# The first layer of block 0 in two 256-token sets, the first of them beside the second half of block 0's attention

## The reference

```python
# attention: batch 4, 8 heads, 768 steps, head size 48; w is the decay of every step
for t in range(S):
    cur = einsum('bhd,bhe->bhde', u * k[t], v[t])
    y[t] = einsum('bhd,bhde->bhe', r[t], state + cur)
    state = w[t][:, :, :, None] * state + einsum('bhd,bhe->bhde', k[t], v[t])
x = y.transpose(0, 2, 1, 3).reshape(3072, 384)
# first layer, d_ff 1536
x = (sigmoid(x @ w_gate) * (x @ w_val)) @ w_out
# second layer, d_ff 2048
h = x @ w2_in
out = where(h > 0, h, exp(min(h, 0)) - 1) @ w2_out
```

## Time and profile before

| | |
|---|---|
| runs shown | 1202.12, 1203.12, 1210.94 us (median 1203.12) |
| the profiled execution, first to last instruction | 1203.3 us |
| TensorE busy | 1155.1 us, 96% |
| VectorE, ScalarE, GpSimd busy | 669.5, 472.2, 295.5 us |
| mean granted TensorE clock | 0.987 |

### The profile page before, as it was taken

The page is one execution under the profiler, slowest core; times in us unless marked ns, Lnnn a source line. Parts: engine busy times, 40 slices in busy tenths (PEclk is TensorE's granted clock), DMA queues, the critical chain, the costliest instruction groups (busy, mean ns, idle before and its releaser), DMA issues.

```text
span 1203.3 us, 18133 instructions
## 1 busy us (share of the span) xinstructions
PE 1155.1 (96%) x6336; PEld 1006.2 (84%) x6336; DVE 669.5 (56%) x1044; ACT 472.2 (39%) x889; POOL 295.5 (25%) x290
## 2 busy tenths in 40 slices
PE   5778998999999999999999999999999999999999
PEld 4666777888888888888888888889999899899998
DVE  8777868494839393939393933354433334343433
ACT  2433444333333333333333333365544545454543
POOL 5563434143615351535153520000000000000000
PEclk9879998999999999999999999999999999999999
DMA  5451624122312231133204004220100101010000
GB/s 85 80 95 44 106 65 86 40 37 30 54 40 27 38 48 43 20 45 39 53 12 54 0 19 138 66 71 23 52 0 12 40 0 52 0 52 0 26 0 26
DMA packets 153413, 51.80 MB, mean 43 GB/s; under 512 B 126624, under 2 KB 148768, under 8 KB 153376
## 3 DMA queue, kind: packets, MB, share of 16 engines
q1 hardware_dynamic: 153376, 51.33, 21.0%
HBM read 41.88 MB, written 9.44 MB: 43 GB/s over the span
## 4 chain that ended last, share of the span: by engine, by line
PE 82%; DVE 11%; issue 4%; ACT 2%; DMA 0%; POOL 0%; DVEq 0%; SPq 0%; POOLq 0%; ACTq 0%
PE ps L606 21%; PE ps L639 17%; PE ps L631 16%; PE ps L615 10%; PE ps L544 7%; DVE RKW L828 6%; PE ps L560 3%; PE ps L534 3%; PE ps L565 2%; PE ps L573 2%; DVE hl L897 1%; DVE A L853 1%; DVE WS L917 1%; ACT RKW L669 1%; PE ps L581 1%
## 5 line engine op out<-in xcount | busy, mean ns | idle before, releaser
L606 PE MATMUL ps<-xh,WS 128*128 128x512 f32 x864 | 251.3, 408 | 1.6 <-DVE xl L888 1.6
L669 ACT ACTIVATE hh<-work 128x512 fp32r<-128x512 f32 x168 | 106.4, 633 | 287.5 <-DVE work L907 205.5
L544 PEld LDWEIGHTS ps<-RKW 128*128 128x128 f32 x1152 | 157.2, 203 | 59.1 <-DVE RKW L828 38.8
L544 PE MATMUL ps<-RKW 128*128 128x128 f32 x1152 | 167.6, 293 | 34.2 <-DVE RKW L828 34.0
L639 PE MATMUL ps<-WS,hh 128*128 128x384 f32 x768 | 198.0, 339 | 0.5 <-DVE hl L897 0.5
L828 DVE TENSOR_TENSOR RKW<-RKW,WL 64x256 f32<-64x256 f32 x288 | 186.1, 646 | 16.1 <-PE ps L544 13.7
L606 PEld LDWEIGHTS ps<-xh,WS 128*128 128x128 f32 x864 | 155.1, 190 | 30.7 <-issue 1.8
L897 DVE TENSOR_TENSOR hl<-work,hh 128x512 fp32r<-128x512 f32 x168 | 133.0, 791 | 85.3 <-ACT hh L669 84.3
L631 PE MATMUL ps<-xh,WS 128*128 128x512 f32 x576 | 164.2, 397 | 0.0
L615 PE MATMUL ps<-hh,WS 128*128 128x512 f32 x432 | 161.6, 411 | 0.4 <-DVE hl L897 0.3
L934 DVE SCALAR_TENSOR_TENSOR work<-work,ps 128x512 f32<-128x512 f32 x96 | 66.0, 688 | 172.2 <-ACT work L757 172.2
(11 more groups left out here) (67 smaller groups left out, 1324.7 us busy)
## 6 DMA issues: line engine op xcount, KB each, us to landing
nat<-in_w_dram SPq DMA_DIRECT2D x24, 192.0 KB, 3.7
nat<-in_k_dram SPq DMA_DIRECT2D x24, 192.0 KB, 4.8
nat<-in_r_dram SPq DMA_DIRECT2D x24, 192.0 KB, 5.2
V<-in_v_dram SPq DMA_DIRECT2D x24, 192.0 KB, 4.5
x_scratch<-work SPq DMA_DIRECT2D x6, 768.0 KB, 3.5
nat<-x_scratch SPq DMA_DIRECT2D x6, 768.0 KB, 5.2
out_dram<-Yt SPq DMA_DIRECT2D x5, 768.0 KB, 3.9
RKW<-in_moe_w_in_dram SPq DMA_DIRECT2D x16, 192.0 KB, 2.4
```

The lines of the kernel that those rows point to most:

```text
L544: last = mm(bank[b][:, p * P:(p + 1) * P].rearrange("p (e i l) -> p e i l", e=2, l=L), K[:, g, :], Rb[:, :, :, 1, :], start=True, stop=True)
L606: last = mm(ps[:, VAL if val else GATE, :], gate_w(a, val, j, c), xp[b][:, c, :], start=(i == 0 and c == 0), stop=(i == 2 and c == KC - 1))
L669: return nc.scalar.activation(o, i, ACT.Copy)
```

## The change

It concerns block 0 only. `FIRST` becomes the attention of half 0 of block 0 and an `XT` for its 256 tokens. Then comes `HALVES`:

- the first layer of these 256 tokens (all 12 slices, 36 groups, matmuls over 256 columns), with the 24 steps of half 1 of block 0's attention and the `XT` of its 256 tokens spread over all 108 thirds;
- the first layer of the other 256 tokens (again 36 groups over 256 columns), with the 48 steps of block 1's attention spread over 99 thirds, then `XT` of block 1 and `LATE`.

From block 1 on everything runs as before. Layer 1 now counts seven sets rather than six blocks. The six early splits move from the second half of the attention to the steps `L5`, `L6` and `KT` of the first; the 30 others come one after each group of the first set. Of the weight pieces eight are now loaded at the start, ahead of the inputs of half 1: six raw buffers in `work` (two of them over `sig` and `h`, so the first sigmoid waits for the sixth split) and two in the unused half of `Yt`; from piece 8 on the ring of four is used. The loads of block 1's inputs move with the steps that free their buffers.

```diff
-    PARTS = [("a", hf, name, b) for hf in range(HALF) for name in STAGES for b in range(U)]
+    PARTS = [[("a", hf, name, b) for name in STAGES for b in range(U)] for hf in range(HALF)]
...
-    MIXED = []
-    for i, third in enumerate(THIRDS):
-        MIXED.append(third)
-        MIXED += [PARTS[s] for s in range(len(PARTS)) if s * (len(THIRDS) - 3) // len(PARTS) == i]
-    MIXED += [XT] + LATE
-    FIRST = PARTS + [XT]
+    def spread(dense, parts, room):
+        steps = []
+        for i, third in enumerate(dense):
+            steps.append(third)
+            steps += [parts[s] for s in range(len(parts)) if s * room // len(parts) == i]
+        return steps
+    MIXED = spread(THIRDS, PARTS[0] + PARTS[1], len(THIRDS) - 3) + [XT] + LATE
+    FIRST = [(0, *part) for part in PARTS[0]] + [(0, "a", 0, "XT", 0)]
+    HALVES = spread([(0, *third) for third in THIRDS + LATE],
+                    [(0, *part) for part in PARTS[1]] + [(0, "a", 1, "XT", 0)], len(THIRDS + LATE)) + \
+             spread([(1, *third) for third in THIRDS],
+                    [(1, *part) for part in PARTS[0] + PARTS[1]], len(THIRDS) - 3) + \
+             [(1, *XT)] + [(1, *third) for third in LATE]
...
-    EARLY = [len(FIRST) // 2 + 10 + 2 * x for x in range(AHEAD)]
+    EARLY = [FIRST.index((0, "a", 0, name, b)) for name in ("L5", "L6", "KT") for b in range(U)]
...
+    def cols(m):
+        return slice(m * TH, (m + 1) * TH) if isinstance(m, int) and m < HALF else slice(0, TOK)
...
-                    if x >= NR1:
-                        sp.wait_ge(d_wlo, x - NR1 + 1)
-                    dst = raw_w1[:, x % NR1, :]
+                    if x >= NR1 + ONCE:
+                        sp.wait_ge(d_wlo, x - (NR1 + ONCE if x < 2 * NR1 + ONCE else NR1) + 1)
+                    dst = w1_raw(x)
...
-            load_v(0, 1, first=True)
-            load_half(0, 1)
-            load_w1(0, NR1)
+            load_w1(0, NR1 + ONCE)
+            load_half(0, 1)
+            load_v(0, 1, first=True)
+            load_w1(NR1 + ONCE, 2 * NR1 + ONCE)
...
-                        last = mm(ps[:, VAL if val else GATE, :], gate_w(a, val, j, c), xp[b][:, c, :],
+                        last = mm(ps[:, VAL if val else GATE, t], gate_w(a, val, j, c), xp[b][:, c, t],
...
-                        last = mm(ps[:, ACC + i, :], down_w(a, j, i), hp[b][:, j % 2, :],
+                        last = mm(ps[:, ACC + i, t], down_w(a, j, i), hp[b][:, j % 2, t],
...
-            for step in FIRST:
-                attention(0, *step[1:])
-            mixed(0)
+            for n, *step in FIRST + HALVES:
+                if step[0] == "a":
+                    attention(n, *step[1:])
+                else:
+                    layer1(n, *step)
```

More of the change, by code:

```diff
@@ L63, in nth, with att_count, xt_set @@
         return use_of(hf, name, i) + 1
-    ORDER = [(hf, name, i) for hf in range(HALF) for name in STAGES for i in range(2)] + \
-            [(0, "XT", i) for i in range(KC)]
-    AT = {use_of(*x): x for x in ORDER}
+    USES = [(hf, name, i) for hf in range(HALF) for name in STAGES for i in range(2)]
+    ORDER = USES + [(0, "XT", i) for i in range(KC)]
+    ORDER0 = USES[:ATT] + [(0, "XT", i) for i in range(KC)] + USES[ATT:] + [(1, "XT", i) for i in range(KC)]
+    assert KC % NBK == 0 and ATT % NBK == 0
+    def att_count(n, hf, name, i):
+        if isinstance(n, int) and n == 0:
+            return ORDER0.index((hf, name, i)) + 1
+        return ATT_BLK * n + KC + nth(hf, name, i)
+    def xt_set(n, hf):
+        return hf if isinstance(n, int) and n == 0 else n + 1
+    TH = U * P
+    def cols(m):
+        return slice(m * TH, (m + 1) * TH) if isinstance(m, int) and m < HALF else slice(0, TOK)
     GROUPS = []
@@ L157, in build @@
         v_loaded = [sem(f"v_loaded{i}") for i in range(HALF)]
-        w1_loaded = [sem(f"w1_loaded{i}") for i in range(NR1)]
+        w1_loaded = [sem(f"w1_loaded{i}") for i in range(N1)]
         w2_loaded = [sem(f"w2_loaded{i}") for i in range(NR)]
@@ L576, in attention @@
                 else:
-                    pe.wait_ge(d_y, 4 * (n + 1))
+                    by_half = isinstance(n, int) and n == 0
+                    pe.wait_ge(d_y, 2 * (hf + 1) if by_half else 4 * (n + 1))
                     for c in range(KC):
                         bank_free(n, hf, name, c)
-                        for b in range(B):
+                        for b in range(hf * U, (hf + 1) * U) if by_half else range(B):
                             last = nc.tensor.transpose(bank[c][:, b * P:(b + 1) * P],
@@ L650, in mixed @@
                     else:
-                        layer1(i, *step)
+                        layer1(i + 1, *step)
             pe.wait_ge(p_const, 1)
-            for step in FIRST:
-                attention(0, *step[1:])
-            mixed(0)
+            for n, *step in FIRST + HALVES:
+                if step[0] == "a":
+                    attention(n, *step[1:])
+                else:
+                    layer1(n, *step)
             with pe.Fori(1, NB - 1) as i:
@@ L659, in _ @@
             for step in LAST:
-                layer1(NB - 1, *step)
+                layer1(NB, *step)
             with pe.Fori(0, NB) as i:
@@ L773, in _ @@
             nc.scalar.activation(first[:], ident[:, 0:1], ACT.Sigmoid)
-            for s, step in enumerate(FIRST):
-                attention(0, *step[1:])
-                if s in EARLY:
-                    split_w1(EARLY.index(s))
-            x = AHEAD
-            for step in MIXED:
+            x = 0
+            for s, (n, *step) in enumerate(FIRST + HALVES):
                 if step[0] == "a":
-                    attention(1, *step[1:])
+                    attention(n, *step[1:])
                 else:
-                    layer1(0, *step)
-                    if step[-1] == 2 and x < N1:
-                        split_w1(x)
-                        x += 1
+                    layer1(n, *step)
+                if s in EARLY or (step[0] != "a" and step[-1] == 2 and x < N1):
+                    split_w1(x)
+                    x += 1
             assert x == N1
@@ L955, in _ @@
             nc.vector.reduce_sum(odd[:], ident[:, 1:P:2], axis=AX.X).then_inc(d_zero, 1)
-            for s, step in enumerate(FIRST):
-                attention(0, *step[1:])
-                if s in EARLY:
-                    split_w1(EARLY.index(s))
-            x = AHEAD
-            for step in MIXED:
+            x = 0
+            for s, (n, *step) in enumerate(FIRST + HALVES):
                 if step[0] == "a":
-                    attention(1, *step[1:])
+                    attention(n, *step[1:])
                 else:
-                    layer1(0, *step)
-                    if step[-1] == 2 and x < N1:
-                        split_w1(x)
-                        x += 1
+                    layer1(n, *step)
+                if s in EARLY or (step[0] != "a" and step[-1] == 2 and x < N1):
+                    split_w1(x)
+                    x += 1
+            assert x == N1
             with dve.Fori(1, NB - 1) as i:
```

164 lines of the change are left out of this document (87 added, 77 removed).

## The result

| | before | after |
|---|---|---|
| median | 1202.62 us (1199.83 to 1210.94) | 1219.99 us (1217.65 to 1220.78) |
| ratio | | 1.0121, 95% interval 1.0085 to 1.0157 |
| span of the profiled execution | 1203.3 us | 1218.1 us |

The change makes the kernel slower by 1.2%. The span grew by 14.8 us, where I had forecast 4 us less.

The account below looks back on a forecast made before the run. VectorE was taken to bound the first stages in the L phase, TensorE everything elsewhere. Stages of 52.6 + 78 + 95.4 = 226 us replace 230.15, with nothing changed after: 1203.3 - 4 = 1199 us, range 1183 to 1213.

Parts of the forecast that it names:

- After it nothing changes: Stages from block 1's layer on: stay at 121.8 us each, 120.7 of them TensorE's.
- Stage A: Attention of half 0 alone, before layer 1: 6.9 + 41.6 + 2.0 + 2.1 = 52.6 us, instead of 94.1.
- Rival 3: Both half sets: 256-column matmuls at 133 ns, 10 us more, 1204 us in all; inside the forecast's range, no separate chance.
- Stage B: First set beside half 1's attention: 17 + 43.5 + 17.5 = 78 us (70 to 84).
- SyncE's queue: Loads of block 1's inputs ahead of weight pieces 29 to 35: 0 us, or 3 us if the pieces land late.
- standstill between product and split: First set's L phase: VectorE waits while ScalarE makes h's high part before copying; 5.8 times 0.85 us, 4.9 us.
- L phase: Attention from first to end of last R scaling: 43.5 us in Stage B, 25.8 per half in Stage C.
- T phase: Attention from first transpose to first R scaling: 17 us in Stage B, 10 per half in Stage C.
- Stage C: Second set beside block 1's attention: two halves 90.4 us plus 5 for the end, 95.4 us (88 to 103).
- end phase: Stage C, from last R scaling to next transpose: 9.4 us instead of 11.85, its eight thirds being half as long.
- Rival 2: Stages B and C: TensorE's granted clock falls to 0.80, 17.5 us more, 1221 us in all; chance 12%.
- Rival 1: Queues smooth Stage B to 71 and Stage C to 86 us, 1183 in all; 26% including cases between it and forecast.

Follow-up runs that it names:

- e5: Changed kernel with the edits of e3 and e4 and 76 filler instructions on TensorE that move the loop's end to .15 of a code piece: 1203.82 us, 1.0007.
- e1: Changed kernel with 119 do-nothing instructions ahead of TensorE's work, putting the loop's end at .32 of a code piece as in before: 1217.79 us, 1.0105.
- e2: Kernel before with 137 do-nothing instructions ahead of TensorE's work, putting the loop's end at .85 of a code piece as in after: 1221.27 us, 1.0146.
- e3: Changed kernel with weight pieces 29 to 34 loaded between the loads of block 1's inputs: 1214.91 us, one run.
- e4: Changed kernel with ScalarE copying the weight piece before it makes the high part of h at each value group: 1215.56 us, one run.
- e11: e5 with the low parts of weight pieces 6 to 35 left out (results not those of the reference): 1192.99 us, one run.
- e8: Kernel before with only ScalarE's order turned round at value groups, piece copy ahead of the high part of h: 1196.76 us, 0.9961.
- e12: e8 with the low parts of weight pieces 6 to 35 left out (results not those of the reference): 1189.68 us, one run.
- e7: Changed kernel with e5's loop position and, in the second set, three times as many thirds ahead of L steps as of others: 1209.50 us, one run.
- e6: e5 without its ScalarE order; GpSimd makes the low parts of the ten weight pieces at value groups: 1205.70 us, 1.0013.
- e9: Kernel before with 60 do-nothing instructions ahead of TensorE's work, putting the loop's end at .55 of a code piece: 1204.34 us, one run.

## Why the prediction was wrong, by its own steps

| step | forecast | after | e5 |
|---|---|---|---|
| layer 1 begins | 52.6 | 52.62 | 53.69 |
| set 0 | 78 (70 to 84) | 82.9 | 75.2 |
| set 1 | 95.4 (88 to 103) | 99.8 | 100.6 |
| block 1's layer begins | 226 | 235.32 | 229.47 |
| its distance to before's 229.98 | -4 | +5.3 | -0.5 |
| the loop, against before | 0 | +9.4 | +0.1 |

**The step that failed is "After it nothing changes: the later stages have 121.8 us each".** It is half of the miss, 9.4 of the 18.8 us between the forecast span (1203.3 - 4) and the measured 1218.1; without it the span would be 1208.7 us. The other half lies in stages B and C, +4.9 and +4.4 us. The loop's work is indeed unchanged; what is new in it are the standstills at its jumps and the lower clock behind the third. That code written out ahead of a loop moves the loop in TensorE's program (from 9.19 to 11.72 here) was no part of my list of what an edit can touch. Shown: e1 and e2, in both directions. Argued only: that the code fetched behind the loop's end pushes the loop's first piece out.

**Stage A was right.** 52.6 and 52.62 us; that the two agree so closely is luck in part: `XT` began at 50.09 us where the terms give 50.5, and from there it took 2.5 us instead of 2.1. The matmuls of 256 columns were, too:

```profile
52.62 0.59 PE L643 MATMUL ps<-xh,WS 128*128 128x256 f32 x3 [1.02 <-DVE xl L928]
...
53.85 0.87 PE L643 MATMUL ps<-xh,WS 128*128 128x256 f32 x6
54.56 0.40 PE L643 MATMUL ps<-xl,WS 128*128 128x256 f32 x2
```

Six start within 54.56 - 53.85 = 0.71 us, 118 ns each where I took 117. Rival 3 is out: no run shows its 133 ns. The trace has two matmuls for each fp32 matmul of attention (in before 1152 at line 544, where the program has 576), and those of 96 columns follow each other at 112 ns, of which 96 columns at 0.459 ns are 44; that the rest is the loading of weights was my estimate.

**Stage B: mechanism partly right, one term put at nothing.** +4.9 us. SyncE's queue was a term of 0, with 3 us if pieces 29 to 35 land late; they land late, and it is about 3.1 us (e3). The eight loads took 7.7 us to issue (100.89 to 108.62), as I had put them. What the term left out is the landing of the first piece behind them, in the chain in order of time

```profile
108.67 4.04 DMA work<-in_moe_w_out_dram
```

so the pieces in the ring had to cover nearly 12 us, and covered about 8 (ScalarE was free for the next at 109.31).

The standstill between product and split was forecast at 0.85 us each and is 0.90:

```profile
117.80 0.56 DVE L958 TENSOR_TENSOR WS<-work,WS 128x384 fp32r<-128x384 f32 x1 [0.90 <-ACT WS L708]
```

The L phase has five of them, 4.5 us (4.9 forecast), and the whole set ten; e4 gave 4.3 us of these 9 back. The phases: T 18.5 instead of 17, L 45.3 instead of 43.5, rest 19.1 instead of 17.5. The late pieces lie in the L phase, which without them would be shorter than forecast; what the T phase and the rest have too much, 3.1 us together, no run explains. What I had wrong is whom TensorE waits for: its gate and value groups wait for their weights (10.4 us), not its L matmuls for R. That VectorE's splitting binds the stage holds (e11). The prediction's first reading holds too, that the 14.2 us by which the first mixed stage of before exceeds a steady one are the splitting: ScalarE's order took away 8.7 of them (e8, a part of it by the clock), and without the low parts the stage is at 121.73 us (e12).

**Stage C: a term mis-sized.** +4.4 us. T 10.7, L 24.4, end 11.6, T 9.9, L 27.0, and from there 16.3 to block 1's layer, against 10, 25.8, 9.4, 10, 25.8 and 9.4 + 5. The L phases, which I took for the risk, were right in the sum (51.4 and 51.6). The end phase is not bound by what I shortened: from 170.50 to 182.14 TensorE is busy without a gap, and 104 instructions less the 68 of `KT`, `Y` and `S` are 36, so 12 thirds, where I had put eight. The missing four are 4 x 3 x 0.117 = 1.4 of the 2.2 us. The same shows in the last stretch, 16.27 of 16.28 us busy. e7 gave 2.2 us of this back and left the R waits (10.7 to 10.2); what else would shorten set 1 wasn't tried.

**Rival 2, the clock, is out as the cause.** It was my slower case, and its 1221 us is close to the result by chance: it needed a clock under 0.92 in the two stages, and they have 0.94 and 0.97 (0.90 in the L phase of set 0 alone, from 71.1 to 116.5 us). Rival 1, smooth queues (B 71, C 86), didn't come about in any run with all the splits in it; e11 has B at 64.9, but C at 99.4.

**What the change is worth.** Without refetch and late loads, and with ScalarE's better order, 1.0007 (e5): nothing. The forecast of 4 us less is near that, but e5 isn't the kernel that was forecast, and the sum (226) is 3.5 us short of e5's 229.5 even with ScalarE's order, which the sum doesn't have. Starting layer 1 at 52.6 instead of 94.1 us hands 41.5 us forward, and both sets pay it back: attention's steps, which are bound by VectorE in the L phases, have half as much matmul work beside them. One set with ScalarE's order (e8) is ahead of two sets with it (e5) by 8.2 us of span, 7.1 by the medians.

## What to carry to other kernels

Code that is added ahead of a loop can slow the loop down (here by 9.4 us over its four passes, e1 and e2): count TensorE's instructions in front of it and in it, and read the page's line of the instruction queue, before and after; if the transfers grow with the number of passes, move the loop. Before starting a stage earlier, look for the short fix in the wait that it is meant to cover: here one operation of ScalarE in front of another gave 0.4%, where the reordering of a whole block gave nothing. When other loads are moved in front of a stream, its buffers have to cover their issuing and the landing of the first piece behind them (7.7 and 4.0 us here). And work that is moved from VectorE to GpSimd isn't off VectorE's time before its other operations have been measured beside it (VectorE's own splits went from 693 to 935 ns, e6).

## What the runs showed of the hardware that I had not expected

- A loop of 1570 TensorE instructions, 6.13 code pieces, runs over its jumps without a refetch (20 to 23 transfers in the whole execution) when it ends at .15, .32, .55 or .70 of a code piece, and is fetched anew on each pass (48 and 50) when it ends at .85. Each refetch costs nine transfers and 2.4 to 4.8 us; the high figures are those of the jumps behind which the granted clock fell to 0.51 and 0.52 for 3 us (after and e2).
- Ten splits on GpSimd (1.02 us each) didn't lower VectorE's busy time in the stage (60.2 us in e3, 60.6 in e6): VectorE's own splits of the same shape went from 693 to 935 ns in the mean.
- A wait that is long met isn't free on TensorE's sequencer: 77 more such instructions (e9 to e2) moved its first matmul from 8.40 to 16.70 us, 108 ns each. As filler for moving code they cost more than the gain unless they stand where TensorE waits anyway (e5).
- In e8 the stage gained twice: the R waits fell by 4.3 us and the granted clock of the stage rose from 0.97 to 1.00, and with it 4.2 us of TensorE's busy time went (126.25 to 122.09). That the shorter waits are what kept the clock up is argued, not shown.
